# Fused attention and two mixture layers in fp32: the sync engine's transfer order, two value roundings and the first product moved

## What is computed

```python
keep = is_sink | in_window                       # 4 sinks, window of 128
scores = np.where(keep, scale * q @ k.T, -1e9)
a = exp(scores - max); a = a / (sum(a) + 1e-9)
x = (a @ v) as [1536, 512]
p = domain_probs / (domain_probs.sum(-1) + 1e-9)
out = sum over e of p[:, e] * (relu(x @ w1[e]) @ w2[e])
h = out @ w_in
result = (h * cos(h)) @ w_out
```

## Time and profile before

| | before |
|---|---|
| median of 3 runs | 842.77 us (842.75 to 843.6) |
| the profiled execution | 842.75 us, of which span 841.0 us |
| TensorE busy | 831.9 us (99%) |
| weight load busy | 743.1 us (88%) |
| GpSimd busy | 558.1 us (66%) |
| VectorE busy | 456.8 us (54%) |
| ScalarE busy | 456.1 us (54%) |
| granted TensorE clock | 1.000 over the span |

### The profile page before, as it was taken

One profiled execution on the slowest core, in us unless ns is written; L12 is line 12 of the kernel. 1 busy time (PEld: TensorE's weight loads), 2 busy tenths in 40 slices (PEclk: granted clock), 3 DMA queues, 4 the chain that ended last, 5 costly groups with the idle time before them and its releaser, 6 DMA issues.

```text
span 841.0 us, 13631 instructions
## 1 busy us (share of the span) xinstructions
PE 831.9 (99%) x4590; PEld 743.1 (88%) x4590; DVE 456.8 (54%) x942; ACT 456.1 (54%) x981; POOL 558.1 (66%) x424
## 2 busy tenths in 40 slices
PE   8999999999999999999999999999999999999998
PEld 6777988988998998998998998998998998998996
DVE  6888723433433438443443333348757759756755
ACT  6698634433423525523523523536857859867863
POOL 4879996475475878565565565978385399685450
PEclk9999999999999999999999999999999999999999
DMA  9774231221131130231131121121120230520202
GB/s 213 173 184 128 76 120 44 89 94 43 65 101 50 51 100 24 78 101 51 51 101 51 51 101 50 52 100 51 51 101 20 82 101 1 177 100 18 84 1 76
DMA packets 73251, 67.29 MB, mean 80 GB/s; under 512 B 40704, under 2 KB 46944, under 8 KB 73184
## 3 DMA queue, kind: packets, MB, share of 16 engines
q1 hardware_dynamic: 73184, 66.42, 25.2%
HBM read 62.96 MB, written 3.19 MB: 79 GB/s over the span
## 4 chain that ended last, share of the span: by engine, by line
PE 88%; POOL 4%; DVE 3%; issue 2%; SPq 1%; DMA 1%; ACT 1%; ACTq 0%; POOLq 0%
PE scores L1414 11%; PE scores L1418 11%; PE scores L1416 11%; PE scores L1446 10%; PE scores L1444 10%; PE scores L1442 10%; PE bank L1444 5%; PE bank L1446 5%; PE bank L1442 5%; PE bank L1414 3%; PE bank L1416 3%; PE bank L1418 3%; DVE x_lo L1078 1%; POOL weights_t L542 1%; DMA probs_in<-in_moe_domain_probs_dram 1%
## 5 line engine op out<-in xcount | busy, mean ns | idle before, releaser
L621 POOL TENSOR_TENSOR w_lo<-w_raw,w_hi 128x512 fp32r<-128x512 f32 x96 | 129.0, 1353 | 158.4 <-ACT w_hi L780 158.3
L1414 PE MATMUL scores<-x_hi,w_hi 128*128 128x384 f32 x528 | 177.7, 337 | 0.6 <-ACT kept L819 0.3
L1418 PE MATMUL scores<-x_hi,w_lo 128*128 128x384 f32 x528 | 176.7, 335 | 0.0
L1416 PE MATMUL scores<-x_lo,w_hi 128*128 128x384 f32 x528 | 176.6, 334 | 0.0
L628 POOL TENSOR_TENSOR w_lo<-w_raw,w_hi 128x1024 fp32r<-128x1024 f32 x48 | 116.2, 2429 | 65.6 <-ACT w_hi L790 65.6
L790 ACT ACTIVATE w_hi<-w_raw 128x1024 fp32r<-128x1024 f32 x48 | 50.8, 1059 | 191.5 <-PE scores L1446 191.5
L1446 PE MATMUL scores<-w_hi,h_lo 128*128 128x512 f32 x384 | 149.8, 390 | 0.0
L1444 PE MATMUL scores<-w_lo,h_hi 128*128 128x512 f32 x384 | 149.7, 390 | 0.0
L1442 PE MATMUL scores<-w_hi,h_hi 128*128 128x512 f32 x384 | 149.4, 389 | 0.0
L1179 DVE SCALAR_TENSOR_TENSOR acc<-scores,probs,acc 128x512 f32<-128x512 f32 x56 | 41.8, 749 | 116.5 <-PE scores L1446 116.5
L1414 PEld LDWEIGHTS scores<-x_hi,w_hi 128*128 128x128 f32 x528 | 99.1, 188 | 2.5 <-issue 1.7
(11 more groups left out here) (131 smaller groups left out, 1555.2 us busy)
## 6 DMA issues: line engine op xcount, KB each, us to landing
w_raw<-in_moe_w_dram SPq DMA_DIRECT2D x30, 1024.0 KB, 5.0
w_raw<-in_moe_w_in_dram SPq DMA_DIRECT2D x8, 1024.0 KB, 5.0
w_raw<-in_moe_w_out_dram SPq DMA_DIRECT2D x8, 1024.0 KB, 5.1
v_nat<-in_v_dram SPq DMA_DIRECT2D x12, 256.0 KB, 3.6
norm<-routing_dram SPq DMA_DIRECT2D x24, 128.0 KB, 3.2
out_dram<-acc SPq DMA_DIRECT2D x12, 256.0 KB, 4.3
k_nat<-in_k_dram SPq DMA_DIRECT2D x11, 256.0 KB, 3.6
q_nat<-in_q_dram SPq DMA_DIRECT2D x11, 256.0 KB, 3.8
```

The costliest lines, as they stand in the source:

```text
L621: nc.gpsimd.tensor_tensor(w1_slots(w1_lo, h % 2, part), w1_part(h % 2, part), w1_slots(w1_hi, h % 2, part).bitcast(F32), ALU.subtract)\
L1414: nc.tensor.matmul(target[:, 0:HALF], w1_hi[:, i, slot, d], x_hi[:, n - 1, d], start=first and d == 0, stop=False, skip_group_check=True)
L1416: nc.tensor.matmul(target[:, 0:HALF], w1_hi[:, i, slot, d], x_lo[:, n - 1, d], start=False, stop=False, skip_group_check=True)
L1418: last = nc.tensor.matmul(target[:, 0:HALF], w1_lo[:, i, slot, d], x_hi[:, n - 1, d], start=False, stop=d == 1, skip_group_check=True)
```

## The change

There are four edits.

- **SP's loop** runs to t = 13. `load_norm(t - 2)` now stands in the same iteration as `store_inverse(t - 2)`, ahead of `load_values(t)`; before, it came as the first thing of the next iteration, behind `load_values(t)`. `load_first(1)`, the up weights of stage 1, now stands between `store_inverse(10)` and `load_norm(10)`, with `store_inverse(11)` and `load_norm(11)` behind it.
- **The down weights of stage 0** (four DMAs of 256 KB) are issued in iterations 5 and 6 instead of 9 and 10.
- **`round_values`** is taken from GpSimd and done by ScalarE, as a copy at the end of rounds 3 and 6. `lower_values(0)` moves on GpSimd from round 0 to round 3.
- **`product(0, 1)`** moves on TensorE behind `turn_weights(23)`.

```diff
-            for t in range(1, T + 1):
-
-                if t >= 3:
-                    load_norm(t - 3)
+            for t in range(1, T + 2):
                 if 5 <= t + 3 < T:
                     load_keys(t + 3)
-                if t >= 2:
+                if 0 <= t - 2 < T:
                     store_inverse(t - 2)
                 if 5 <= t + 3 < T:
                     load_queries(t + 3)
+                if t == T:
+                    load_first(1)
+                if 0 <= t - 2 < T:
+                    load_norm(t - 2)
                 if 3 <= t < T:
                     load_values(t)
-                if t % TPB == 1:
+                if t % TPB == 1 and t < T:
                     place_sinks(t // TPB)
-                if t in (9, 10):
-                    load_parts(w2_raw, 1, 2 * (t - 9), w2_landed)
-            store_inverse(T - 1)
-            load_first(1)
-            load_norm(T - 2)
-            load_norm(T - 1)
+                if t in (5, 6):
+                    load_parts(w2_raw, 1, 2 * (t - 5), w2_landed)
+
             load_second(1)
...
-            def round_values(b):
-
-                pool.wait_ge(v_diagonal_made, 2 * b + 2)
-                nc.gpsimd.tensor_copy(v_sink[0:HS, b], v_diagonal[:]).then_inc(v_sink_hi_ready, 1)
...
                     spread_values(0)
-                    round_values(0)
-                    lower_values(0)
                 elif i % 2 == 1 and (i + 3) // 2 < T:
                     sink_keys((i + 3) // 2)
+                if i in (3, 8):
+                    lower_values(i // 8)
                 if i == 4:
                     spread_values(1)
-                    round_values(1)
-                elif i == 8:
-                    lower_values(1)
...
+                if i in (3, 6):
+                    b = i // 3 - 1
+                    act.wait_ge(v_diagonal_made, 2 * b + 2)
+                    nc.scalar.activation(v_sink[0:HS, b], v_diagonal[:], ACT.Copy).then_inc(v_sink_hi_ready, 1)
...
-                if i == ND:
-                    pe.wait_ge(masked_ready, NQ)
-                    product(0, 1)
                 if 0 <= i - TURN_LAG < ND:
                     turn_weights(i - TURN_LAG)
...
+                if i == ND:
+                    pe.wait_ge(masked_ready, NQ)
+                    product(0, 1)
                 if i == ND + 1:
```

## The result

| | before | after |
|---|---|---|
| median | 842.8 us (842.75 to 843.81) | 849.78 us (849.27 to 852.99) |
| the profiled execution | 842.75 us, span 841.0 | 849.2 us, span 847.5 |
| ratio of the medians | | 1.0086, 95% interval 1.0066 to 1.0105 |
| mean granted TensorE clock | 1.000 | 0.998 |

The kernel became **7.0 us slower**, 0.86%. The forecast was 843.8 us with a range up to 846.3; it was wrong: the time lies beyond the range, and beyond the 847.3 us of its slow rival too.

The account below looks back on a forecast made before the run. TensorE was taken to bound the kernel, its 24 stages only shifted. 842.75 + 0.8 (first product) + 0.1 (value loads) + 0.1 (down weights) = 843.75, rounded to 843.8 us; range 842.4 to 846.3 us.

Parts of the forecast that it names:

- slow rival: The DMA queue fills up in iterations 5 to 7: 846.3 us, or 847.3 with one full stall; chance 0.22.
- What bounds the kernel: TensorE from 30 us to the end: a microsecond it loses comes out as time; the 24 stages only shift.
- The first product, +0.8: Transposes before stage 0 wait for the exponentials, ending 0.96 us later; stage 0 0.78 us late; bounds 0.68 to 0.96.
- The value loads, +0.1: Iteration 3: value load issued at 32.49 us, landing at 36.1; TensorE waits 0.1 us for tile 3; bounds none to 0.7.
- The down weights, +0.1: Iterations 5 and 6: value tile 7 lands at 61.0 us, 0.5 us of air; loss between 0 and 3 us.
- The rounding on ScalarE, 0: Rounds 3 and 6: two copies of at most 0.60 us cost TensorE nothing; bounds 0 and 0.6 us.
- the end of SP's loop, 0: Last norm loads and `load_second(1)` come some 3 us later, but stage 1's products are 31 us later: 0 us.
- The collision of GpSimd and VectorE: At 23.18 us GpSimd starts within 0.1 us of before; VectorE's 1.20 us instruction stays slow; 1.04 us if it vanished.
- the DMA queue fills up: Early down weights delay iterations 5 to 7; value tile 7 2.5 us late, 846.3 us, or 847.3 with full stall; chance 0.22.

Follow-up runs that it names:

- the kernel with waits of 1.24 us at most: The changed kernel with only the down weights of stage 0 put back into iterations 9 and 10: 846.34 us, ratio 1.0038 [1.0024, 1.0051].

## Why the prediction was wrong, step by step

- **What bounds the kernel: right.** Each wait of TensorE between 30 us and stage 0 came out as time; the stages were only shifted.
- **The first product, +0.8: right in the mechanism, 0.3 us too low.** A wait of 0.9 us at the transposes was foretold, 0.87 and 0.88 us came. Alone it cost 1.1 us [0.4 to 1.9], and 1.2 us in the changed kernel once no value tile was late. Of the part given back at VectorE's wait, nothing came back: that wait grew from 0.28 to 0.5 us, where it should have shrunk to 0.1. So the cost is 0.91 + 0.21 = 1.12 us by the starts, above the prediction's bound of 0.96.
- **The value loads, +0.1: the step that failed.** The prediction took the store's landing as a constant 3.00 us (from one row), saw that a store lands sooner with less ahead of it ("256 KB fewer stand ahead of it") but used that for the same turn only, and let the turn of SP's loop grow only by the value issue, to 5.7 us. But the same exchange puts the value tile and the key tile right ahead of the *next* store. Four stores from 33.25 to 55.57 us took 16.31 us instead of 12.00, +4.31. With the start at 31.98 in place of 32.5 (-0.5), norm issues of 1.24 instead of 1.43 (-0.75) and one value issue of 1.48 us instead of 0.59 (+0.9), the working that gave 57.4 us for value tile 7 gives 61.4; it was 61.48. The turn was 6.8 to 8.5 us from the second on, longer than the 6.4 us that TensorE needs, where the prediction had 0.7 us of air growing tile by tile. Alone the edit cost 2.6 us. TensorE waited just 0.20 us for tile 3, the only one that this step worked out; in the second profiled execution of the changed kernel it was 1.26 us.
- **The down weights, +0.1: failed by the same step.** Their two issues of 1.05 us were counted, their 512 KB ahead of the store were not (4.54 and 4.62 us landings). Alone they cost nothing, since the values then stand ahead of the wait; on top of the norm loads they cost 4 us. The sum was made of edits priced one by one, and the two share one quantity, the turn of SP's loop.
- **The rounding on ScalarE, 0, and the end of SP's loop, 0:** not contradicted. `load_second(1)` was issued at 110.26 us in place of 103.30, 7.0 us later, of which 6.3 are the lateness of the whole kernel there, and TensorE never waited for it. With the early down weights, the two measured 1.0002 [0.9993, 1.0011].
- **The collision of GpSimd and VectorE: wrong, without weight.** The row of 1.20 us became 0.86 us and GpSimd's subtraction came 0.62 us earlier, not within 0.1. It is not the main reason why the changed kernel was 0.62 us ahead at 33 us: VectorE's list was 0.48 us ahead before that row already (L992 at 19.89 us, before L999 at 20.37). What gave the start wasn't found; the rounding alone on the kernel before brought no gain. The gain was lost at the first late value tile, as the prediction said of such a gain.
- **The rival "the DMA queue fills up"** named the place (iterations 5 to 7), the sign and the point from which it decides. Its price, 2.5 us, was too low for two reasons: it began at the down weights, although every store from iteration 4 on was later, and it left the clock at 1.00. What was set against it, that SP waits for its own store every turn and so little stands in the queue, is the error itself: SP waits behind what it has just issued.

The Trainium skill has the rule that the failed step lacked: "DMA: Bandwidth & Descriptors", section "Queues, rings and completion order", says that the descriptors of a queue are consumed in ring order on each DMA engine, and that the increment of a semaphore lands only after every earlier write from that engine. By it a store's completion waits for the loads ahead of it. The runs agree: in iterations 4 to 7 SP went on 0.1 to 0.35 us after the load ahead of the store had landed, the same 4 KB store was complete after 1.24 us with half a value tile 1.8 us ahead and after 4.62 us with 1 MB ahead, and 6 us of the kernel's time hung on its place before or behind a key load. The page gives no price for it; the prediction had used only the page's latencies, for the rival.

## What to carry to other kernels

In this kernel the wait for a small store ended, in most turns, when the load issued just ahead of it had landed (4.62 us with 1 MB ahead, 1.24 us with half a value tile issued 1.8 us ahead); when an edit moves a load, ask which *next* store it now stands in front of, and try the store first (849.8 to 844.1 us here). Price edits that lengthen the same loop together: compare the new turn with the turn of the engine that it feeds, over all iterations, not at the first one. A step whose slack per tile changes sign costs more with each tile.

## What the runs showed of the hardware that was not expected

- The landing of the same 4 KB store, by the tiles that stood ahead of it in the queue: 1.23 to 1.25 us where the value tile ahead had landed or did within 1 us (half tiles 1.8 and 3.1 us ahead, and whole ones 3.1 and 3.3 us ahead in the kernel with the store first); 1.98 us with 256 KB 1.4 us ahead; 2.13 and 2.85 us with 128 and 256 KB right ahead; 3.3 to 3.8 us with a value and a key tile, 4.5 to 4.6 us with the down weights as well. The last two also had a query tile issued right behind, and the two norm loads (128 KB each) stood ahead of the value tile every time. In the second profiled execution of the changed kernel the last two are 3.7 to 4.3 and 4.1 to 4.4 us, so the step from one to the other is within the scatter of single stores.
- The granted clock fell to 0.50 after waits of TensorE of 1.93, 2.53 and 2.66 us for value tile 7, and stayed at 1.00 in the kernel with waits of 1.24 us at most. The length of a wait does not decide by itself: in the two profiled executions with only the product taken back, TensorE also waited 2.74 and 2.63 us for value tile 3, and the clock stayed at 1.00 there. In the changed kernel the lower clock shows for about 4 us and takes 1.6 to 1.7 us of work.
